# Two fused expert layers behind a gated scan: the second layer of chunks 0 and 1 joined into one stage at the end

## The chip, the cores and the metric

The kernel runs on one core of one Trainium2 chip. The metric is the device time of one execution in microseconds; the median of several runs counts. TensorE does the matrix products, ScalarE (ACT) and VectorE (DVE) the element-wise work on fp32 tiles, GpSimd (POOL) more of it, and SyncE (SP) issues the DMAs.

## What is computed

6080 tokens of 256 features run through a gated recurrence and then through two feed-forward layers, in fp32 (x is the scan's output for the first, and the first layer's output for the second):

```python
f = lower_bound + (1.0 - lower_bound) * sigmoid(f_logit)
for t in range(S):                      # the scan
    h = f[:, t] * h + (1 - f[:, t]) * x[:, t]
    y[:, t] = h
h = x @ w_in0                           # 256 -> 2048
x = (h * sigmoid(1.702 * h)) @ w_out0   # 2048 -> 256
h = x @ w_in1
g = where(h >= 1, h, where(h <= -1, 0, (h + 1) ** 2 / 4))
out = g @ w_out1
```

## The kernel before

**Precision.** Each fp32 product is made of three fp32r matmuls: every operand is split into a high part (a rounded copy, made by ScalarE: the functions with `_hi`) and the remainder (a subtraction, made by VectorE or GpSimd: `_lo`), and high x high, high x low and low x high are added up in PSUM (`three`, L566). A matmul has a 128 x 128 stationary operand and a moving one of `width(si)` columns (tokens).

**Stages.** Tokens are cut into seven chunks (L18); a stage `(l, c)` is layer l over chunk c, and the stages run one after another in the order of `STAGES` (L26): (0,0) (0,1) (1,0) (0,2) (1,1) (0,3) (1,2) (0,4) (1,3) and so on to (0,6) (1,5) (1,6), numbered by `si` from 0. Chunks 0 and 1, of 448 and 512 tokens, are plain: 16 tiles (one of 128 hidden features each), and for each tile 6 matmuls up into a hidden bank and 6 down into two accumulators (`unit`, L599, called for d = 0 and 1), so 192 matmuls a stage. Chunks 2 to 6 have 1024 tokens, two times 512, and use a fast scheme with seven block products in place of eight for the first matrix of a layer: 8 groups a stage, each with 7 products of 3 matmuls of 512 columns and 4 units of 6 matmuls, so 45 matmuls (`group`, L702). Between the products of a chain ScalarE takes snapshots of the bank (`take`, L870), which TensorE waits for (s_snap), and VectorE adds them to other banks (`evac`, L1195). Down products of a tile come three tiles (or about a group) behind its up products, so the element-wise work on a tile has about 5 us of slack.

**Inputs of a stage.** A seven-product stage needs seven input tiles (B11, B21, B22, T1, T3, T2, T4; `x_hi`, `x_lo`), among them sums of the others (`t_sum` on VectorE for layer 0, `z_sum` on GpSimd for layer 1). They are made during the stage before. For layer 0 they come from the scan of the chunk (`sigmoid_step` and `f_step` on ScalarE, `drive_step` and `scan_step` on VectorE, in four quarters), whose gate and state are loaded by `load_gate` and `load_state`, 1024 KB each.

**Weights.** The up weights of a layer are split once, in the first stage that uses them (`blocks_hi`, `blocks_lo`), stored in DRAM (`keep_blocks`) and loaded for each later group by `load_weights` (L451), two groups ahead; a seven-product group also needs four sums of blocks (`weight_sums`, `sums_hi`, `sums_lo`, `keep_sums`; job 0 to 7 for layer 0, 8 to 15 for layer 1; where each is made is said by `SUMS_AT`, L185). Its load is three DMAs of 256, 512 and 128 KB, and TensorE waits for all three before the group's first product. The down weights are split once and stay in SBUF (`down_hi`, `down_lo`); their raw form comes through small buffers in zraw, by `load_raw_down`, which waits until the buffer's last user is done.

**Order.** Every engine runs its own program, written out by hand: `plain_fill(si, s)` names the extra work at tile s of a plain stage, `fill(si, g, place)` that in a group. SyncE's program (L514) is one queue: whatever stands behind a waiting instruction waits too.

## Time and profile before

| | us |
|---|---|
| median of 3 runs (1017.29 to 1018.53) | 1017.85 |
| the profiled execution | 1017.41 |
| its span, first to last instruction | 1015.6 |
| TensorE busy | 1007.3 |
| ScalarE busy | 705.0 |
| VectorE busy | 687.6 |
| GpSimd busy | 579.4 |

The span is shorter than the execution's time by what lies around the first and the last instruction. A matmul's row shows how long it was in the pipeline (0.39 us for 512 columns), and the next one begins before it ends: the pitch from start to start is what counts. DMAs are issued by SyncE's queue, and "to landing" is the time from issue to the last byte's signal.

### The profile page before, as it was taken

Reading aid. Unit: us, or ns where it says so; the run is one execution under the profiler, and the core shown is the slowest. Engines: PE = TensorE matmul, PEld = TensorE weight load, DVE = VectorE, ACT = ScalarE, POOL = GpSimd, SP = SyncE. Lnnn points to the kernel's source line nnn. Section 1 sums busy time; section 2 is a strip of 40 time slices with the busy share of each in tenths; the row PEclk is TensorE's granted clock in tenths of the full one; section 3 lists DMA queues with packets and bytes.
Section 4 is the critical chain, followed back from the end, with each engine's and each line's share of the span. In section 5 each row is a group of like instructions: output and inputs, shape, how many; then the busy total and the mean of one; then the engine's idle time right before and its main releaser. Section 6 shows DMA issues by size and latency. Waiting matters only on the chain.

```text
span 1015.6 us, 14155 instructions
## 1 busy us (share of the span) xinstructions
PE 1007.3 (99%) x4401; PEld 821.6 (81%) x4401; DVE 687.6 (68%) x959; ACT 705.0 (69%) x1305; POOL 579.4 (57%) x471
## 2 busy tenths in 40 slices
PE   8999999999999999999999999999999999999998
PEld 6988988888888888888888888888888888888886
DVE  7764766665665786666677667678665546767666
ACT  7666767666766776677677676667766667777665
POOL 4577768756677364456647346745635664673432
PEclk9999999999999999999999999999999999999999
DMA  9766564436523232532223333232324222232421
GB/s 314 249 239 208 178 245 157 145 130 217 192 96 107 73 109 73 179 128 77 106 73 109 145 108 127 83 100 73 109 73 147 77 84 99 73 110 73 149 75 42
DMA packets 53212, 130.76 MB, mean 129 GB/s; under 512 B 6032, under 2 KB 16912, under 8 KB 52112
## 3 DMA queue, kind: packets, MB, share of 16 engines
q1 hardware_dynamic: 52992, 129.85, 36.8%
q8 instruction: 35, 0.57, 0.2%
q14 instruction: 41, 0.34, 0.1%
q10 hardware_dynamic: 144, 0.00, 0.0%
HBM read 106.82 MB, written 23.00 MB: 128 GB/s over the span
## 4 chain that ended last, share of the span: by engine, by line
PE 98%; DVE 0%; DMA 0%; POOL 0%; issue 0%; ACT 0%; SPq 0%; DVEq 0%; POOLq 0%
PE chain L568 26%; PE acc L623 17%; PE acc L620 17%; PE acc L619 17%; PE pair L568 13%; PE single L568 7%; DMA state<-x_dram 0%; POOL w_down0lo L1403 0%; DVE acc L1132 0%; DVE state L1113 0%; SPq L495 0%; ACT xin0hi L802 0%; DVE zout L1192 0%; ACT w_down0hi L852 0%; DVE acc L1098 0%
## 5 line engine op out<-in xcount | busy, mean ns | idle before, releaser
L1443 POOL TENSOR_TENSOR g_lo<-g_act,g_hi 128x512 fp32r<-128x512 f32 (+1 forms) x269 | 355.0, 1321 | 397.0 <-ACT g_hi L915 392.0
L875 ACT ACTIVATE spare<-chain 128x512 f32<-128x512 f32 x240 | 143.3, 597 | 189.5 <-PE chain L568 189.0
L1204 DVE TENSOR_TENSOR spare<-pair,spare 128x512 f32<-128x512 f32 x160 | 110.6, 691 | 181.9 <-PE pair L568 181.5
L915 ACT ACTIVATE g_hi<-g_act 128x512 fp32r<-128x512 f32 (+1 forms) x269 | 168.1, 625 | 5.4 <-DVE g_act L1228 3.4
L568 PE MATMUL chain<-xin1hi,w_main 128*128 128x512 f32 x416 | 162.6, 395 | 0.0
L623 PE MATMUL acc<-g_lo,w_down0hi 128*128 128x512 f32 (+1 forms) x384 | 150.2, 391 | 0.0
L619 PE MATMUL acc<-g_hi,w_down0hi 128*128 128x512 f32 (+1 forms) x384 | 149.8, 390 | 0.3 <-POOL w_down0lo L1403 0.3
L623 PE MATMUL acc<-g_lo,w_down1hi 128*128 128x512 f32 (+1 forms) x384 | 150.0, 391 | 0.0
L620 PE MATMUL acc<-g_hi,w_down1lo 128*128 128x512 f32 (+1 forms) x384 | 149.9, 390 | 0.0
L620 PE MATMUL acc<-g_hi,w_down0lo 128*128 128x512 f32 (+1 forms) x384 | 149.9, 390 | 0.0
L619 PE MATMUL acc<-g_hi,w_down1hi 128*128 128x512 f32 (+1 forms) x384 | 149.7, 390 | 0.0
L568 PE MATMUL chain<-xin0hi,w_main 128*128 128x512 f32 (+2 forms) x360 | 134.5, 385 | 0.1
L908 ACT ACTIVATE g_act<-g_act,one_half 128x512 f32<-128x512 f32 (+1 forms) x96 | 68.7, 716 | 63.4 <-DVE g_act L1215 63.4
L1204 DVE TENSOR_TENSOR single<-single,spare 128x512 f32<-128x512 f32 x80 | 55.7, 697 | 60.0 <-PE single L568 59.6
L568 PEld LDWEIGHTS chain<-xin1hi,w_main 128*128 128x128 f32 x416 | 78.1, 188 | 18.4 <-DMA w_a<-blocks_kept 0.3
L619 PEld LDWEIGHTS acc<-g_hi,w_down0hi 128*128 128x128 f32 x384 | 72.0, 188 | 16.9 <-POOL w_down0lo L1403 0.4
L619 PEld LDWEIGHTS acc<-g_hi,w_down1hi 128*128 128x128 f32 x384 | 72.1, 188 | 16.7
L620 PEld LDWEIGHTS acc<-g_hi,w_down1lo 128*128 128x128 f32 x384 | 72.0, 188 | 16.7
L620 PEld LDWEIGHTS acc<-g_hi,w_down0lo 128*128 128x128 f32 x384 | 72.0, 188 | 16.5
L623 PEld LDWEIGHTS acc<-g_lo,w_down0hi 128*128 128x128 f32 x384 | 72.1, 188 | 16.1 <-DVE g_lo L1239 0.3
L623 PEld LDWEIGHTS acc<-g_lo,w_down1hi 128*128 128x128 f32 x384 | 72.1, 188 | 15.6
L568 PE MATMUL chain<-xin1lo,w_main 128*128 128x512 f32 x208 | 82.2, 395 | 0.0
(126 smaller groups left out, 1960.6 us busy)
## 6 DMA issues: line engine op xcount, KB each, us to landing
w_main<-sums_kept SPq DMA_DIRECT2D x80, 512.0 KB, 3.6
w_main<-blocks_kept SPq DMA_DIRECT2D x80, 256.0 KB, 2.8
w_a<-blocks_kept SPq DMA_DIRECT2D x80, 128.0 KB, 3.9
blocks_kept<-w_main SPq DMA_DIRECT2D x16, 512.0 KB, 4.3
w_main<-blocks_kept SPq DMA_DIRECT2D x16, 512.0 KB, 3.3
sums_kept<-xin0hi SPq DMA_DIRECT2D x16, 512.0 KB, 2.9
zout<-w_in_dram SPq DMA_DIRECT2D x24, 256.0 KB, 4.3
out_dram<-zout SPq DMA_DIRECT2D x10, 512.0 KB, 5.3
```

The source lines that it names most:

```text
L568: mm = pe.matmul(to, w[a], moving[b], start=start and i == 0, stop=stop and i == 2, skip_group_check=joined)
L619: pe.matmul(to, w[0], g_hi[i][:, 0:n], start=start, stop=False)
L620: pe.matmul(to, w[1], g_hi[i][:, 0:n], start=False, stop=False)
L623: pe.matmul(to, w[0], g_lo[i][:, 0:n], start=False, stop=stop).then_inc(s_unit, 1)
L875: act.activation(snap[k][:, 0:n], chain[g % 2][:, 0:n], ACT.Copy).then_inc(s_snap, 1)
L908: act.activation(t, t, ACT.Square, bias=one_half[:], scale=0.5).then_inc(s_t, 1)
L915: act.activation(g_hi[h % 4][:, 0:n], activated(h), ACT.Copy).then_inc(s_ghi, 1)
L1204: dve.tensor_tensor(to[:, 0:n], bank[:, 0:n], snap[(0, 2, 1)[k]][:, 0:n], ALU.add).then_inc(s_evac, 1)
L1443: pool.tensor_tensor(g_lo[h % 4][:, 0:n], g_act[h % 4][:, 0:n], g_hi[h % 4][:, 0:n].bitcast(F32), ALU.subtract).then_inc(s_glo_pool, 1)
```

## The change

The second layer of chunks 0 and 1 is no longer done in two plain stages (448 and 512 tokens, 384 matmuls). The 960 tokens are taken together as a chunk of two times 480, in seven products, and are the last stage, `(1, JOINED)`. The first layer's results for chunks 0 and 1 are stored in DRAM (`keep_z`) and loaded again one stage before the last (`load_z`).

The order of stages becomes (0,0) (0,1) (0,2) (0,3) (1,2) (0,4) (1,3) (0,5) (1,4) (0,6) (1,5) (1,6) (1,7): 13 stages, so that (0,2) follows (0,1) at once, and (0,3) follows (0,2). All inputs of (0,2) are made in stage 1 (ScalarE at tiles 7 to 13, GpSimd at `X_LO_AT`), and all eight `down_lo` of layer 1 too, by VectorE at `DOWN_AT`, where GpSimd did four of them. Since no plain stage of layer 1 is left, the blocks of layer 1 aren't made in place any more, but in jobs of their own ahead of the sums (`more_hi`, `more_lo`, `keep_more`), in stages 2, 3 and 4 (`SUMS_AT`: jobs 8 and 9 in groups 4 and 5 of stage 2, 10 and 11 in groups 0 and 1 of stage 3, 12 to 15 in groups 0 to 3 of stage 4). There they share one buffer, so each waits for the store of the one before. The sums' buffers move from xin0hi to zout and raw_more. TensorE waits for each input tile of a stage by itself instead of for the last of them, and in the first group after a plain stage the single product and a unit come before the second product of the chain. The core of the diff:

```diff
-WIDTH = (448, 512, 512, 512, 512, 512, 512)
-CHUNKS = len(WIDTH)
+WIDTH = (448, 512, 512, 512, 512, 512, 512, 480)
+CHUNKS, JOINED = 7, 7
 PLAIN = 2
 SPAN = [n if c < PLAIN else 2 * n for c, n in enumerate(WIDTH)]
 BASE = [K * P * sum(SPAN[:c]) for c in range(CHUNKS + 1)]
-assert sum(SPAN) == TOKENS
-STAGES = [(0, 0), (0, 1), (1, 0)]
-for _c in range(2, CHUNKS):
-    STAGES += [(0, _c), (1, _c - 1)]
-STAGES += [(1, CHUNKS - 1)]
+OUT_BASE = {c: 0 if c == JOINED else BASE[c] for c in (JOINED, *range(PLAIN, CHUNKS))}
+assert sum(SPAN[:CHUNKS]) == TOKENS and sum(SPAN[:PLAIN]) == SPAN[JOINED]
+STAGES = [(0, 0), (0, 1), (0, 2), (0, 3)]
+for _c in range(4, CHUNKS):
+    STAGES += [(1, _c - 2), (0, _c)]
+STAGES += [(1, CHUNKS - 2), (1, CHUNKS - 1), (1, JOINED)]
...
 for _g in range(4):
-    SUMS_AT[1, 4 * _g + 1] = _g
-for _g in range(3):
-    SUMS_AT[4, 2 * _g + 1] = NG + 3 + _g
-for _g in range(7):
-    SUMS_AT[3, _g] = 4 + _g
+    SUMS_AT[1, 3 * _g + 1] = _g
+    SUMS_AT[2, _g] = 4 + _g
+    SUMS_AT[4, _g] = NG + 4 + _g
 for _g in range(2):
-    SUMS_AT[5, _g] = 2 * NG - 2 + _g
+    SUMS_AT[2, 4 + _g] = NG + _g
+    SUMS_AT[3, _g] = NG + 2 + _g
+LATE = {3: 1, 5: 0, 7: 0}
+X_LO_AT = (8, 9, 11, 12, 13, 14, 15)
+DOWN_AT = (0, 2, 4, 6, 8, 13, 14, 15)
...
+        z_kept = nc.dram_tensor("z_kept", (P, K, SPAN[JOINED]), F32, kind="Internal").ap()
...
-        made_sums = [xin[0][0][:, 2 + 2 * r:4 + 2 * r, :].rearrange("p a b -> p (a b)") for r in range(2)]
+        made_sums = [zout[:, 0:1024].bitcast(F32R), raw_more[:].bitcast(F32R)]
...
+                if SUMS_AT.get((4, job - NG - 4)) == job and job < NG + 6:
+                    sp.wait_ge(s_xlo, input_n(4, 6))
...
+            def keep_more(job):
+                sp.wait_ge(s_more, job - NG + 1)
+                sp.dma_start(blocks[job], made_sums[0].bitcast(F32)).then_inc(s_kept_blocks[job - NG], 16)
+            def keep_z(si):
+                n, m = WIDTH[si], 2 * BANK[si]
+                for d in range(K):
+                    sp.wait_ge(s_z[d], evac_n(si, 0))
+                begin = sum(WIDTH[:si])
+                sp.dma_start(z_kept[:, :, begin:begin + n], zraw[:, m * n:(m + K) * n].rearrange("p (d n) -> p d n", d=K))\
...
+            def load_z():
+                n = WIDTH[JOINED]
+                sp.wait_ge(s_z_kept, 32)
+                sp.wait_ge(s_xlo, input_n(NS - 2, 6))
+                for t in range(2):
+                    sp.dma_start(zraw[:, t * K * n:(t + 1) * K * n].rearrange("p (d n) -> p d n", d=K),
+                                 z_kept[:, :, t * n:(t + 1) * n]).then_inc(s_z_back, 16)
...
-                    if g in (2, 4, 6):
-                        load_raw_down(1, g // 2 + 1)
-                    if g in (4, 5):
-                        load_raw_up(1, 2 * (g - 4))
-                        load_raw_up(1, 2 * (g - 4) + 1)
-                if si == 2:
-                    keep_blocks(1, g)
-                    if g + 4 < NG:
-                        load_raw_up(1, g + 4)
-                    if g in (0, 1, 5):
-                        load_raw_down(1, (5, 6, 0, 0, 0, 7)[g])
+                    if g < 5:
+                        load_raw_down(1, g + 2)
+                    if g == 5:
+                        keep_z(0)
+                    if g == 6:
+                        load_raw_down(1, 7)
+                        load_gate(3)
+                if (si, g) == (2, 0):
+                    load_state(3)
+                if (si, g) == (2, 2):
+                    keep_z(1)
+                if (si, g) == (3, 0):
+                    load_gate(4)
+                    load_state(4)
+                if (si, g) == (3, 7):
+                    load_raw_sums(12)
+                    load_raw_sums(13)
+                if (si, g) == (NS - 2, 0):
+                    load_z()
                 if not is_plain(si):
+                    if SUMS_AT.get((si, g), 0) >= NG:
+                        keep_more(SUMS_AT[si, g])
                     kept(si, g)
...
+                if g == 0:
+                    pe.wait_ge(s_xlo, input_n(si, xs))
...
+                if si == 4 and start and d == 0:
+                    pe.wait_ge(s_down_dve, down_made(1, NG - 1)[1])
...
+                if after_plain and g == 0:
+                    half_unit(second, 0)
                 pe.wait_ge(s_snap, third_n(S, 0))
                 product(si, g, S2, T2, c, False).then_inc(s_chain, 1)
-                half_unit(second, 0)
-                if first is not None:
-                    single_product(si, g)
+                if not (after_plain and g == 0):
+                    half_unit(second, 0)
+                    if first is not None:
+                        single_product(si, g)
...
+            def more_hi(job):
+                act.wait_ge(s_raw_sums[job % 2], 16 * (job // 2 + 1))
+                if job == NG:
+                    act.wait_ge(s_kept_sums[NG - 2], 16)
+                else:
+                    act.wait_ge(s_kept_blocks[job - NG - 1], 32)
+                act.activation(made_sums[0].rearrange("p (a b f) -> p a b f", a=4, b=2)[:, :, 0, :],
+                               raw_sums[job % 2].rearrange("p (a f) -> p a f", a=4), ACT.Copy).then_inc(s_more_hi, 1)
...
+                if job < 2:
+                    blocks_made(act, NG - 1)
+                elif job < NG:
+                    act.wait_ge(s_kept_sums[job - 2], 16)
+                elif job == NG:
+                    act.wait_ge(s_kept_sums[NG - 1], 16)
+                else:
+                    act.wait_ge(s_kept_sums[job - NG - 1], 32)
...
+                    act.wait_ge(s_tsum, tsum_n(si, T4))
+                    act.wait_ge(s_xlo, input_n(si, (T1, T3, T2)[k]))
...
+                    if s == 7:
+                        z_evac(0, 0)
+                    for j in {7: (B11,), 8: (B21,), 10: (B22,), 11: (T1,), 12: (T3, T2), 13: (T4,)}.get(s, ()):
+                        x_hi(2, j)
+                    if s in DOWN_AT:
+                        down_hi(1, DOWN_AT.index(s))
...
+                if SUMS_AT.get(following, 0) >= NG:
+                    more_hi(SUMS_AT[following])
...
+            def more_lo(job):
+                dve.wait_ge(s_more_hi, job - NG + 1)
+                made = made_sums[0].rearrange("p (a b f) -> p a b f", a=4, b=2)
+                dve.tensor_tensor(made[:, :, 1, :], raw_sums[job % 2].rearrange("p (a f) -> p a f", a=4),
+                                  made[:, :, 0, :].bitcast(F32), ALU.subtract).then_inc(s_more, 1)
...
+                    if s in (6, 8):
+                        drive_step(2, 2 + s // 8)
+                    if s == 9:
                         last_scan(2)
-                    if s in (7, 8):
-                        direct_lo(s - 7)
-                if si == 2:
-                    if s == 4:
-                        z_evac(1, 0)
-                    if s in (3, 5, 7):
-                        t_sum(3, s // 2 - 1)
-                    if s in (1, 8, 10, 12):
-                        down_lo(1, {1: 4, 8: 5, 10: 6, 12: 7}[s])
-                if si == 4:
-                    if s == 1:
-                        last_scan(3)
-                    if s in (3, 4):
-                        z_evac(3, s - 3)
-                    if s in (8, 10, 12):
-                        t_sum(5, (s - 8) // 2)
+                    if 10 <= s <= 12:
+                        t_sum(2, s - 10)
+                    if s in DOWN_AT:
+                        down_lo(1, DOWN_AT.index(s))
...
+                if place == 0 and SUMS_AT.get((si, g), 0) >= NG:
+                    more_lo(SUMS_AT[si, g])
+                if si == 2:
+                    if 1 <= g <= 4 and place == 0:
+                        drive_step(3, g - 1)
+                    if 1 <= g <= 3 and place == 2:
+                        scan_step(3, g - 1)
+                    if (g, place) == (4, 2):
+                        last_scan(3)
+                    if (g, place) in ((4, 3), (5, 0), (5, 2)):
+                        t_sum(3, {(4, 3): 0, (5, 0): 1, (5, 2): 2}[g, place])
...
+                    if late and (g, place) == (0, 3):
+                        drive_step(c, 3)
+                    if (g, place) == (late, 1):
+                        last_scan(c)
...
+                    if STAGES[si][1] == JOINED:
+                        pool.wait_ge(s_z_back, 32)
+                    else:
+                        for d in range(K):
+                            pool.wait_ge(s_z[d], evac_n(STAGES.index((0, STAGES[si][1])), 1))
+                    if si == 4:
+                        pool.wait_ge(s_kept_blocks[SUMS_AT[3, 1] - NG], 32)
+                    else:
+                        pool.wait_ge(s_store, stored_n(si - 2))
...
+                    if s in X_LO_AT:
+                        x_lo(2, X_LO_AT.index(s))
...
```

## Rows read from the trace of the kernel before

**Rows 1.** The page: busy us, share, instructions; then the granted clock in 40 slices.
```profile
PE 1007.3 (99%) x4401; PEld 821.6 (81%) x4401; DVE 687.6 (68%) x959; ACT 705.0 (69%) x1305; POOL 579.4 (57%) x471
...
PEclk9999999999999999999999999999999999999999
```

**Rows 2.** The chain that ended last: start us, us, what; TensorE's first products of tiles and groups.
```profile
18.33 1.23 PE chain L568 x6
...
42.77 1.23 PE pair L568 x6
...
77.92 1.38 PE single L568 x6
...
80.68 1.37 PE chain L568 x6
...
88.98 1.23 PE single L568 x6
...
294.24 0.71 PE chain L568 x3
...
315.12 0.71 PE chain L568 x3
```

**Rows 3.** The timeline of SyncE in stage 1: start us, us, engine, line, what.
```profile
76.56 0.33 SPq L458 DMA_DIRECT2D w_main<-blocks_kept  x1
```

**Rows 4.** The timeline of ScalarE and of VectorE at tile 12 of stage 1.
```profile
79.82 0.62 ACT L915 ACTIVATE g_hi<-g_act 128x512 fp32r<-128x512 f32 x1
...
79.96 0.70 DVE L1222 SCALAR_TENSOR_TENSOR single<-g_act,single 128x512 f32<-128x512 f32 x1 [1.48 <-ACT g_act L901]
```

**Rows 5.** Groups by shape: line, engine, op, out<-in, count | busy us, mean ns | idle before.
```profile
L1113 DVE SCALAR_TENSOR_TENSOR state<-gate,state 128x512 f32<-128x512 f32 x20 | 20.9, 1044 | 0.0
...
L1132 DVE TENSOR_TENSOR_SCAN state<-gate,state 128x512 f32<-128x512 f32 x10 | 15.1, 1511 | 0.0
...
L1184 DVE TENSOR_TENSOR w_down1lo<-zraw,w_down1hi 128x512 fp32r<-128x512 f32 x4 | 5.1, 1273 | 0.6 <-ACT w_down1hi L852 0.6
...
L1170 DVE TENSOR_TENSOR spare<-state 128x1024 f32<-128x1024 f32 x2 | 2.8, 1424 | 0.0
```

**Rows 6.** The timeline of VectorE and of GpSimd (POOL) at tile 7 of stage 1.
```profile
63.97 2.32 DVE L1132 TENSOR_TENSOR_SCAN state<-gate,state 128x512 f32<-128x512 f32 x1
...
63.92 1.28 POOL L1443 TENSOR_TENSOR g_lo<-g_act,g_hi 128x512 fp32r<-128x512 f32 x1 [0.29 <-ACT g_hi L915]
```

**Rows 7.** Windows: us, then busy us of PE, PEld, DVE, ACT, POOL, granted clock, DMA share, GB/s.
```profile
116.00:119.00 3.00, 3.00 (x16) 2.76 (x16) 2.56 (x4) 1.72 (x5) 2.88 (x3) 1.00 0.89 369
61.32:88.98 27.66, 27.66 (x121) 22.52 (x121) 16.81 (x24) 16.26 (x31) 21.09 (x21) 1.00 0.55 188
...
367.17:377.60 10.43, 10.43 (x47) 8.45 (x46) 10.01 (x12) 8.13 (x17) 7.38 (x6) 1.00 0.24 87
```

**Rows 8.** SyncE's issues, and landing of the gate (issued 112.83) and state (issued 131.20) loads.
```profile
111.89 0.33 SPq L434 DMA_DIRECT2D blocks_kept<-w_main  x1
...
DMA to landing us min/median/max: 5.9/5.9/5.9
...
129.82 0.32 SPq L461 DMA_DIRECT2D w_main<-blocks_kept  x1
...
DMA to landing us min/median/max: 7.5/7.5/7.5
```

**Rows 9.** Timelines of VectorE and ScalarE in group 2 of a seven-product stage of layer 1.
```profile
359.01 0.69 DVE L1204 TENSOR_TENSOR spare<-pair,spare 128x512 f32<-128x512 f32 x1 [1.48 <-PE pair L568]
...
363.19 0.60 ACT L875 ACTIVATE spare<-chain 128x512 f32<-128x512 f32 x1 [1.09 <-PE chain L568]
...
366.55 0.72 ACT L908 ACTIVATE g_act<-g_act,one_half 128x512 f32<-128x512 f32 x1 [0.72 <-DVE g_act L1215]
```

**Rows 10.** The timeline of TensorE in the head; in brackets its idle time before.
```profile
3.37 3.71 PE L760 MATMUL pair<-warm 128*128 128x512 bf16 x9 [3.37 <-ACT gate L788]
7.86 0.37 PE L568 MATMUL single<-xin0hi,w_main 128*128 128x224 f32 x1 [0.78 <-POOL w_main L1380]
```

More of the change, by code:

```diff
@@ L691, in plain_stage @@
                         first_up(1, s).then_inc(s_up, 1)
-                    if before is False and s < 4:
-                        for d in range(K):
-                            unit(h0 - 4 + s, d)
-                    elif before and s < LAG:
+                    if si == 1 and s < LAG:
                         for d in range(K):
@@ L1409, in x_lo @@
                 if plain:
[L1410 removed]
+                    tile = column(source, 2 + j, n)
                 else:
```

364 lines of the change are left out of this document (136 added, 228 removed).

## The prediction

> **What bounds the kernel now.** First the page's busy shares and slices: TensorE is busy for 1007.3 of 1015.6 us, and the granted clock is at nine tenths or more in every slice [rows 1]. Then the chain of work that ended last: behind the head it is made of matmuls, and the same step recurs at a fixed pitch: 24.44 us for ten tiles of 12 matmuls in a plain stage of 448 tokens, 11.06 us for four in one of 512, and 20.88 us for two groups (90 matmuls) in a seven-product stage [rows 2]. Last the waits of TensorE itself: 3.37 and 0.78 us in the head [rows 10], and beyond that only tenths. So time is the number of matmuls times their pitch, plus head and tail, and a part of the change counts if it alters that number, or if it makes a wait on TensorE where there is none.
>
> **The change, part by part.** All sums are made against the profiled execution, 1017.41 us with a span of 1015.6; it lies 0.44 under the median of 1017.85, which is inside the spread of the three runs.
>
> *Matmuls removed.* A plain stage has 16 tiles of 12 matmuls, a seven-product stage 8 groups of 45. Per matmul the pitches are 24.44/120 = 0.2037 us (448 columns), 11.06/48 = 0.2304 (512) and 20.88/90 = 0.232 (512, seven products) [rows 2]; 64 columns cost 0.0267 us, so 0.42 ns each, and 480 columns in a seven-product stage cost 0.232 - 32 x 0.00042 = 0.2186. Out go 192 x 0.2037 = 39.11 and 192 x 0.2304 = 44.24 us, in come 360 x 0.2186 = 78.70. That is 83.35 - 78.70 = 4.65, or **4.7 us** (5.1 if the 480-column matmul takes the plain stage's overhead). The moved stages keep their matmuls. Nothing at the old boundaries is saved, since no boundary had an idle TensorE. The last evacuation and store are 480 wide instead of 512: under 0.1 us, left out.
>
> *The new third stage waits for its weights.* This is the largest cost. In stage 1 tiles 12 and 13 begin at 77.92 and 80.68, tiles 14 and 15 follow at the same pitch, and the next stage's first matmul stands at 88.98 [rows 2]. Stages 0 and 1 keep their matmuls, so this is when (0,2) wants its weights. In the new order SyncE, at group 6 of stage 1, first issues load_raw_down(1, 7), which waits until VectorE has done down_lo(1, 5) at tile 13, since they share a buffer; then load_gate(3), 1024 KB; and only then the 896 KB of the first group's weights. SyncE gets to group 6 just after it has issued the weights for group 7, which it did at 76.56 [rows 3]; nothing else holds it up before.
> When does down_lo(1, 5) end? ScalarE begins the copy behind tile 12's tanh at 79.82 and takes 0.62 us [rows 4]; x_hi(2, T4) and down_hi(1, 5) follow at 0.5 to 0.6 us each, so the copy is there at about 81.5, and the subtraction takes 1.27 us [rows 5]: 82.8 at the earliest. It can't be much earlier, since on VectorE it is behind tile 12's gate step of 79.96 to 80.66 [rows 4]. It can be later: VectorE gets, in tiles 6 to 12 (19.4 us), seven gate steps and four remainders of 0.7, two drives of 1.04, two down_lo of 1.27, two scans of 1.5 to 2.3, and three T sums, of which the double one takes 1.42 and the single ones, taken as two thirds to all of it, 1.0 to 1.4 [rows 5, 6]: 18.7 to 21.2 us. And there the two engines hinder each other: a scan, 1.5 us in the mean, took 2.32 beside a GpSimd subtraction that had begun 0.05 before it and took 1.28 [rows 6]. GpSimd, busy for 21.1 of 27.7 us in that stretch [rows 7], gets seven x_lo where it had three down_lo and a blocks_lo. I take 84.0, between 82.8 and 85.5.
> How long do the transfers take? In a like case 512, 256 and 1024 KB were issued at 111.89, 112.44 and 112.83, and the last landed 5.9 us after its issue, so 6.8 us for 1792 KB [rows 8], while the DMA engines moved up to 369 GB/s [rows 7]. Here 256, 1024 and 896 KB stand in the queue: 384 KB more, 1.1 us: 8.0. In another case 896 KB and then 1024 KB took from 129.82 to 131.2 + 7.5 = 138.7, 8.9 us for 1920 KB, which with the 256 KB more gives 9.6 here [rows 8]. I take 8.4, nearer to the first, where nothing else was queued. So the weights land at 84.0 + 8.4 = 92.4 against 88.98: **3.4 us** of idle TensorE (bounds 82.8 + 8.0 and 85.5 + 9.6: 1.8 to 6.1). Should GpSimd be late with a remainder in stage 1, TensorE waits there instead and this wait shrinks by as much, so I don't add it.
> The slowdown of VectorE beside GpSimd is stated by the Trainium skill (SBUF — State Buffer, "Who interferes with whom"): whichever of the two starts first on the shared port pair holds it for its whole instruction. The 2.32 us scan agrees. By that rule taken strictly, the seven x_lo and VectorE's operations with two SBUF inputs would add up end to end in stage 1, and the wait would be near its upper bound.
>
> *Weights of layer 1 made in stages 2 to 4.* Per job ScalarE gets one more copy (0.6), VectorE a subtraction of about 1.27, SyncE a 512 KB store. The room in a layer-1 group: ScalarE waits 1.09 us ahead of its third snapshot, and behind it 0.72 for VectorE [rows 9]. Between the product that a snapshot follows and the product that needs it TensorE has two or three others of 3 matmuls, 1.4 to 2.1 us, of which the snapshot takes 0.6; so ScalarE may be about 1 us late at a snapshot before TensorE feels it. VectorE has a hole of 1.48 us behind a group's first gate step [rows 9], just where more_lo is put; but in group 3 of a layer-1 stage it is busy for 10.0 of 10.4 us [rows 7], and in stage 4 it now gets more_lo in each of groups 0 to 3, and in group 1 the last scan. I expect 0.3 us there (0 to 2). In stage 2, group 4, VectorE has more_lo, a drive, a scan and a T sum beside the regular work: by the same durations over 11 us of work in 10.44, spread over two groups: 0.2 (0 to 1). At the start of stage 3 the gate and state of chunk 4, 2048 KB, are issued ahead of the store of keep_more(10), which more_hi(11) waits for on ScalarE: at the rate above it lands about 11 us into a group of 10.44, and ScalarE's takes of group 1 stand behind that wait: 0.4 (0 to 1.5). Together **0.9** (0 to 4); not below nothing, since TensorE doesn't idle there now.
>
> *Free edits.* Storing z of chunks 0 and 1 and reloading it (four transfers of about 0.5 MB) lies in stages 1, 2 and 11; the reload is issued at the start of the stage before its use, where a group's stretch moves 87 GB/s [rows 7]. The direct copies from the accumulator go; they were hidden. Eight groups of blocks are no longer made in place in (1,0). Uncovered, each would cost under 1 us. The end has three layer-1 stages in a row; the inputs of the last are made in the same places as before, with the store of two stages back as the only new wait of GpSimd, which it has in every mid stage.
>
> **Sum.** 1017.41 - 4.7 + 3.4 + 0.9 = 1017.0.
>
> **Rivals.**
> (B) *The gain arrives.* The wait for weights is at its lower bound or under it, and the rest is absorbed: 1017.41 - 4.7 + 1.8 = 1014.5; down to 1012.7 if there is no wait at all. For: the slack of about 5 us between a tile and its second-layer unit, which hid all such work so far. Against: the queue order can't be undone by a quick engine, since the copy and the subtraction of tile 13 stand behind tile 12.
> (C) *The clock falls in the wait.* The idle time is long, 5 us, and the granted clock drops to 1.2 GHz for a stretch. The nine first matmuls, after an idle head of 3.37 us, took 3.71 us for 9 x 512 columns [rows 10], 0.41 us each, the pace of 1.2 GHz (the granted clock in the slices is too coarse to show it [rows 1]), against 0.23 later: that costs 3.71 - 9 x 0.23 = 1.6 us. 1017.41 - 4.7 + 5.0 + 0.9 + 1.6 = 1020.2. It is slower than before from a total loss of 4.7 us, and measurably so from 6.8. For: VectorE and GpSimd hold each other up in the very tiles that gate the load. Against: a wait of 0.78 us in the head was followed by the full pace (224 columns every 0.11 us), so only a long wait can do it [rows 10].
> The Trainium skill says the same of long gaps (TensorE: Matmul & The Clock Gate, "HAM oscillation"): a DMA wait that is long enough sends the clock back to half, and it is paid anew at each such wait. No stretch of this trace after the head shows it.
> (D) *The joined stage doesn't run at TensorE's pace*, because fixed costs of the other engines don't shrink with 480 columns: 0.1 us per group, 1017.8. Against: ScalarE is busy for 8.1 of 10.4 us in such a group, and VectorE's 10.0 hold T sums [rows 7] that the last stage lacks.
>
> **How the numbers follow.** Forecast 0.48 (1015.8 to 1019.5), B 0.29, C 0.18, D and what I don't see 0.05. A measurement can tell about 0.2%, 2.0 us, from no change: that is under 1015.8 or over 1019.9. B gives faster 0.29; C and the upper edge of the forecast and D slower 0.23; the rest 0.48. The range of 8 in 10 takes in most of B and of C: 1013.6 to 1020.8; the forecast's own is 1015.8 to 1019.5.
>
> **What would show it.** 4377 matmuls instead of 4401, the last stage's groups at about 9.84 us. At about 89 us one idle stretch of TensorE, ended by a DMA into w_main or w_a, whose issue stands behind that of gate, behind a wait of SyncE for w_down1lo. Short gaps before the snapshots' products in stages 2, 3 and 4. The forecast is wrong if TensorE goes through 89 us without a pause, or if a gap of over 1 us appears elsewhere.

## The result, and the profile after

The changed kernel takes **1028.67 us** (median of 5, 1027.53 to 1029.47), the one before 1017.85 beside it: a ratio of 1.0106, 95% interval 1.0091 to 1.0121. It is slower by 10.8 us, where the forecast was 1017.0 with a range that ended at 1020.8. The profiled execution took 1029.47, with a span of 1027.7 against 1015.6. (It is the longest of the five; the difference of its span, 12.1 us, is therefore 1.2 us more than that of the medians.)

The page of the changed kernel: busy us, share and instructions; the granted clock in 40 slices; and the shares of the chain that ended last.
```profile
PE 1010.1 (98%) x4377; PEld 819.5 (80%) x4377; DVE 707.4 (69%) x985; ACT 719.4 (70%) x1334; POOL 596.5 (58%) x476
...
PEclk9998999999999999999999999999999999999999
...
PE 88%; POOL 3%; DMA 3%; issue 2%; ACT 2%; DVE 1%; SPq 0%; ACTq 0%; DVEq 0%; POOLq 0%
```
The 24 matmuls are gone (4401 in [rows 1]). But the fourth slice of the clock shows an 8, and 12% of the chain now lie outside TensorE (2% before). Where it stood is read from TensorE's timeline: the first matmul behind each wait has its idle time in brackets.

TensorE's timeline in the changed kernel: start us, us, what, idle before and what ended it.
```profile
88.79 0.40 PE L676 MATMUL acc<-g_lo,w_down0hi 128*128 128x512 f32 x1
93.18 0.80 PE L617 MATMUL chain<-xin0hi,w_main 128*128 128x512 f32 x1 [4.00 <-DMA w_a<-blocks_kept]
93.78 0.63 PE L617 MATMUL chain<-xin0lo,w_main 128*128 128x512 f32 x1
94.20 0.63 PE L617 MATMUL chain<-xin0hi,w_main 128*128 128x512 f32 x1
...
139.78 0.64 PE L617 MATMUL chain<-xin0hi,w_main 128*128 128x512 f32 x1 [2.17 <-ACT spare L916]
140.21 0.63 PE L617 MATMUL chain<-xin0lo,w_main 128*128 128x512 f32 x1
...
194.41 0.50 PE L617 MATMUL chain<-xin1hi,w_main 128*128 128x512 f32 x1 [0.54 <-ACT spare L916]
...
197.64 0.51 PE L672 MATMUL acc<-g_hi,w_down0hi 128*128 128x512 f32 x1 [0.58 <-DVE zraw L1215]
...
302.89 0.50 PE L617 MATMUL chain<-xin0hi,w_main 128*128 128x512 f32 x1 [1.35 <-ACT spare L916]
...
957.83 0.37 PE L617 MATMUL chain<-xin0hi,w_main 128*128 128x480 f32 x1
...
967.66 0.38 PE L617 MATMUL chain<-xin0hi,w_main 128*128 128x480 f32 x1
...
977.49 0.37 PE L617 MATMUL chain<-xin0hi,w_main 128*128 128x480 f32 x1
```
Behind the waits of 4.00 and 2.17 us the matmuls begin 0.43 us apart, not 0.23: that is the half clock (1.2 GHz). Windows of the same kernel show it beside what the DMA engines moved.

Windows: us, then busy us of PE, PEld, DVE, ACT, POOL, granted clock, DMA share, GB/s.
```profile
92.20:99.03 6.83, 5.85 (x14) 4.60 (x15) 0.32 (x1) 1.11 (x2) 2.81 (x5) 0.50 1.00 406
99.10:105.00 5.90, 5.90 (x25) 4.48 (x25) 1.84 (x4) 4.14 (x8) 0.14 (x1) 1.00 0.00 0
...
139.99:143.40 3.41, 3.41 (x9) 2.66 (x9) 3.41 (x4) 0.74 (x2) 3.41 (x3) 0.50 0.39 155
```
The account of the span. A gap's loss is the distance between the starts of the two matmuls around it less the usual pitch; the clock's is 0.2 us for each matmul in a half-clock stretch (14 and some 8 of them, at 0.427 against 0.232; in the first 1.0 of the 6.8 us TensorE was still idle).

| where | us |
|---|---|
| matmuls removed | -4.7 |
| start of stage 2, at 89 to 93: idle | +4.1 |
| the half clock behind it, 6.8 us of it | +2.7 |
| stage 2, at 137 to 140: idle | +2.3 |
| the half clock behind it, 3.4 us of it | +1.6 |
| start of stage 3, at 194 to 198: four small gaps | +1.9 |
| stage 4, at 282 to 314: gaps of 0.6, 0.65, 1.6 and 0.7 | +3.6 |
| small ones at 85, 101, 136 and 144 | +1.1 |
| sum (measured: 12.1) | +12.6 |

The mean granted clock of the profiled execution is 0.995, that of the four others 0.997 or 0.998, so they had less of the half clock than the table shows.

### The profile page after: what moved, and what is told of

It is laid out like the page before. It is cut to its first block, busy times and chain, and to the rows that moved or that the text cites. A ratio compares the mean times of both kernels' runs of the same rounds, so it can differ in the third digit from the quotient of the medians.

```text
span 1027.7 us, 14282 instructions
## 1 busy us (share of the span) xinstructions
PE 1010.1 (98%) x4377; PEld 819.5 (80%) x4377; DVE 707.4 (69%) x985; ACT 719.4 (70%) x1334; POOL 596.5 (58%) x476
## 4 chain that ended last, share of the span: by engine, by line
PE 88%; POOL 3%; DMA 3%; issue 2%; ACT 2%; DVE 1%; SPq 0%; ACTq 0%; DVEq 0%; POOLq 0%
PE chain L617 24%; PE acc L676 16%; PE acc L672 16%; PE acc L673 16%; PE pair L617 11%; PE single L617 6%; DMA blocks_kept<-zout 1%; POOL g_lo L1470 1%; DMA zout<-w_in_dram 1%; DMA w_a<-blocks_kept 1%; POOL xin1lo L1438 1%; ACT g_hi L956 0%; POOL raw_more L1418 0%; POOL xin0lo L1438 0%; DVE zout L1182 0%
## 5 line engine op out<-in xcount | busy, mean ns | idle before, releaser
L1470 POOL TENSOR_TENSOR g_lo<-g_act,g_hi 128x512 fp32r<-128x512 f32 (+2 forms) x277 | 367.9, 1330 | 400.9 <-ACT g_hi L956 392.4
L916 ACT ACTIVATE spare<-chain 128x512 f32<-128x512 f32 (+1 forms) x264 | 156.8, 594 | 203.5 <-PE chain L617 196.7
L1227 DVE TENSOR_TENSOR spare<-pair,spare 128x512 f32<-128x512 f32 (+1 forms) x176 | 120.9, 687 | 185.6 <-PE pair L617 185.3
L956 ACT ACTIVATE g_hi<-g_act 128x512 fp32r<-128x512 f32 (+2 forms) x277 | 172.9, 624 | 4.2 <-DVE g_act L1251 3.3
L617 PE MATMUL chain<-xin0hi,w_main 128*128 128x512 f32 (+3 forms) x424 | 163.8, 390 | 8.2 <-DMA w_a<-blocks_kept 4.0
L617 PE MATMUL chain<-xin1hi,w_main 128*128 128x512 f32 x352 | 137.8, 395 | 0.5 <-ACT spare L916 0.5
L1227 DVE TENSOR_TENSOR single<-single,spare 128x512 f32<-128x512 f32 (+1 forms) x88 | 61.1, 695 | 69.8 <-PE single L617 69.6
L617 PEld LDWEIGHTS chain<-xin0hi,w_main 128*128 128x128 f32 x424 | 80.0, 189 | 27.2 <-ACT spare L916 5.7
L1238 DVE TENSOR_SCALAR g_act<-spare 128x512 f32<-128x512 f32 (+1 forms) x96 | 87.1, 907 | 3.3
```

What stands on the lines that cost most here:

```text
L617: mm = pe.matmul(to, w[a], moving[b], start=start and i == 0, stop=stop and i == 2, skip_group_check=joined)
L916: act.activation(snap[k][:, 0:n], chain[g % 2][:, 0:n], ACT.Copy).then_inc(s_snap, 1)
L956: act.activation(g_hi[h % 4][:, 0:n], activated(h), ACT.Copy).then_inc(s_ghi, 1)
L1227: dve.tensor_tensor(to[:, 0:n], bank[:, 0:n], snap[(0, 2, 1)[k]][:, 0:n], ALU.add).then_inc(s_evac, 1)
L1238: dve.tensor_scalar(g_act[i][:, 0:n], hidden_of(h), -1.0, 1.0, ALU.max, ALU.min).then_inc(s_clip, 1)
L1470: pool.tensor_tensor(g_lo[h % 4][:, 0:n], g_act[h % 4][:, 0:n], g_hi[h % 4][:, 0:n].bitcast(F32), ALU.subtract).then_inc(s_glo_pool, 1)
```

## The first wait: what stands in the queue of SyncE

The theory of the prediction (Q below): the wait at 89 is set by the order of SyncE's queue, since the first weights of stage 2 stand behind `load_raw_down(1, 7)`, which waits for VectorE, and behind the 1024 KB of `load_gate(3)`. The rival (V): VectorE, ScalarE and GpSimd have so much to do in stages 1 and 2 that TensorE would wait for them anyway. SyncE's issues in the changed kernel:
```profile
76.44 0.56 SPq L499 DMA_DIRECT2D w_main<-blocks_kept  x1
84.04 0.34 SPq L440 DMA_DIRECT2D zraw<-w_out_dram  x1
84.43 0.42 SPq L408 DMA_DIRECT2D gate<-f_logit_dram  x1
84.96 0.36 SPq L502 DMA_DIRECT2D w_main<-blocks_kept  x1
85.37 0.43 SPq L504 DMA_DIRECT2D w_main<-sums_kept  x1
85.84 0.60 SPq L508 DMA_DIRECT2D w_a<-blocks_kept  x1
```
SyncE stands still from 77 to 84.04, and the last of the three weight transfers (`w_a`, 7.3 us from issue to landing) is there at 93.14.

**Both loads out of the way.** They go behind the weights:
```diff
-                    if g == 6:
-                        load_raw_down(1, 7)
-                        load_gate(3)
...
                 if G + 2 < GROUPS and not is_made(G + 2):
                     load_weights(G + 2)
+                if (si, g) == (1, 6):
+                    load_raw_down(1, 7)
+                    load_gate(3)
```

> At group 6 of stage 1 SyncE issues the 896 KB of weights for (0,2) first, and load_raw_down(1, 7) and load_gate(3) behind them. Theory Q (the queue's order makes the wait): the weights are issued at about 82.2 us and land by 86, the idle 4.1 us at 93 us goes, and with it the fall of the clock behind it (3.4 us): 1028.7 - 7.5 = 1021.2. Rival V (ScalarE, VectorE and GpSimd are late in stage 1 and TensorE would wait for their input tiles in any case): the gap only changes its releaser, at least 3 us of it stay, and the clock may still fall: 1025 or more. The gaps at 140, 194 and 282 to 314 us stay in both.

Measured: median 1025.34 (4 runs, ratio 1.0062, 1.0041 to 1.0083), the profiled execution 1022.02 with a span of 1020.2, 7.5 less than 1027.7, as Q says. The gap of 4.1 us became two, 0.6 at 92 to 95 and 0.6 at 103, and no clock fell in that trace. But the three other executions took 2.7 to 4.6 us longer than the profiled one, at mean granted clocks of 0.998 and 0.999, and the median is only 3.3 us under that of the changed kernel, inside V's range. What those executions lost isn't shown. So it is the trace that speaks for Q here, not the median; two kernels that differ in this wait alone follow below (`e10_first_wait`).

**One at a time.** `e2_gate_behind` moves `load_gate(3)` alone, `e3_raw_behind` `load_raw_down(1, 7)` alone.

> Only load_gate(3) goes behind the weights; the wait for down_lo(1, 5) stays ahead. Q, with both causes needed: the weights are issued at 84.5 and land 4.5 to 5 us later, at 89 to 89.5, so the gap shrinks to 0.5 us and the clock stays up: 7 us off a profiled execution of about 1028. If the wait for VectorE alone is the cause, over 2 us of the gap stay; by V at least 3.

> Only load_raw_down(1, 7) goes behind the weights; the 1024 KB of gate stay ahead. Q, with both causes needed: nothing holds SyncE up, gate is issued at about 77 and the weights at 82.2, landing by 86.5: no gap at 93 us, no fall of the clock there, 7.5 us less. If the bytes alone are the cause, over 2 us of the gap stay; by V at least 3.

Measured: 1025.17 (span 1023.4) and 1022.31 (span 1020.5), one execution each, so that only their traces are read. With the gate behind, TensorE still waits for weights, but shortly:
```profile
91.59 0.50 PE L618 MATMUL chain<-xin0hi,w_main 128*128 128x512 f32 x1 [0.96 <-DMA w_a<-blocks_kept]
```
With the raw block behind, it doesn't wait at all between 88 and 94 (0.27 us at 94.5, 0.58 at 103). So the whole gap needs VectorE's wait: without it the 1024 KB cost nothing, since the gate load is then issued at 77.92, 4.5 us ahead of the weights. While that wait stands, the 1024 KB make up about 2.9 of the 4.1 us, and 1.2 stay without them.

## Stages 2 and 3: the engine that waits in order

In stage 2 ScalarE comes late to the snapshot that TensorE needs at 139.78. ScalarE's timeline in the changed kernel, there and at the start of stage 3:
```profile
134.46 0.63 ACT L894 ACTIVATE raw_more<-zout 128x512 fp32r<-128x512 f32 x1 [2.40 <-POOL zout L1413]
136.97 0.63 ACT L874 ACTIVATE zout<-zout 128x512 fp32r<-128x512 f32 x1 [1.88 <-DMA zout<-w_in_dram]
...
139.15 0.57 ACT L916 ACTIVATE spare<-chain 128x512 f32<-128x512 f32 x1
...
192.21 0.63 ACT L874 ACTIVATE zout<-zout 128x512 fp32r<-128x512 f32 x1 [3.14 <-DMA blocks_kept<-zout]
...
193.79 0.58 ACT L916 ACTIVATE spare<-chain 128x512 f32<-128x512 f32 x1
```
L874 is `more_hi`, L916 a snapshot. At 137 `more_hi(8)` waits for its raw load, which was issued only at 131.98; the snapshot stands behind it. At 192 `more_hi(11)` waits for the store of job 10, issued at 182.08 behind 2048 KB, 10.0 us from issue to landing. Two edits, first both together, on top of the first experiment:
```diff
-    SUMS_AT[2, 4 + _g] = NG + _g
+    SUMS_AT[2, 5 + _g] = NG + _g
...
-                if (si, g) == (3, 0):
-                    load_gate(4)
-                    load_state(4)
                 if not is_plain(si):
                     if SUMS_AT.get((si, g), 0) >= NG:
                         keep_more(SUMS_AT[si, g])
                     kept(si, g)
+                if (si, g) == (3, 0):
+                    load_gate(4)
+                    load_state(4)
```

> Three moves together: weights first as in e1; jobs 8 and 9 one group later (groups 5 and 6 of stage 2), so that the raw weights of each have landed before the copy that needs them; and at the start of stage 3 the store of keep_more(10) ahead of load_gate(4) and load_state(4). If ScalarE's waits for DMAs are the cause of the gaps at 140 us (2.3 us, and 1.7 for the clock) and 194 us (1.95), these go as well: 1028.7 - 7.5 - 4.0 - 1.9 = 1015.3. If they come from too much work on VectorE, GpSimd and ScalarE there, the same gaps turn up one group later, and the time stays at 1019 or more.

Measured: median 1017.80 (10 runs, ratio 0.9999, 0.9989 to 1.0008), span 1016.3. The gaps in stage 2 and at 190 are gone, with nothing left of either. What is left: 1.35 us at 92 to 95, 0.6 at 103, and 3.5 in stage 4. The median is 2.5 us above the 1015.3 that was expected. Against `e1_weights_first` it is 7.5 us less, where the spans differ by 3.9: again what the usual execution of that kernel lost isn't shown.

Each alone, on the changed kernel, so with the first wait still in it:

> The changed kernel with one edit: the first two weight jobs of layer 1 (8 and 9) in groups 5 and 6 of stage 2, not 4 and 5. In its trace ScalarE waited 1.88 us for the raw load of job 8 and 2.40 for the sums in group 4, TensorE lost 2.3 us at 139.8 and the granted clock was half for 3.4 us. If that load's place is the cause, this gap and this fall of the clock go (about 4 us less span, 1023.7) and the gaps at 93 and 194 stay; if the work of jobs 8 and 9 is just too much for stage 2, the gap moves one group on.

> The changed kernel with one edit: at the start of stage 3 the store of job 10 is issued ahead of the gate and state of chunk 4 (2048 KB). In its trace the store took 10.05 us from issue to landing, ScalarE waited for it until 192.2, and TensorE lost 1.95 us at 194 to 198. If what is in flight ahead of the store is the cause, that gap goes to under 0.3 us and the span falls by 1.7 to 2.0, with the gaps at 93 and 140 as they were. If two splits, two sums and their remainders in two groups are the cause, at least 1 us of it stays.

Measured: 1025.82 (span 1024.0) and 1024.77 (span 1023.0), one execution each. With the jobs later the gap at 140 and its half clock are gone, and 1.4 of the 1.9 us at 190 stay. With the store first the gaps at 194 are gone, and in stage 2 1.0 and 1.6 us are lost at 137 and 141, but the clock stays up there. Its span fell by 4.7 us, of which only the 1.9 at 194 are the edit's; most of the rest is that the half clock lasted 3.4 us behind the first wait, not 6.8, and didn't come at 140. Each edit removes its own gap, and neither gap moved on to another group.

The trace of `e5_store_first`, whose stage 2 is that of the changed kernel, shows a second cause there. ScalarE waited for the raw load for only 0.20 us, and still TensorE was idle for 0.49 and 1.37. The second time the snapshot waited for VectorE, which had `more_lo` (L1182) and a drive step (L1134) ahead of the addition (L1227) that ScalarE needed:
```profile
136.66 1.78 DVE L1182 TENSOR_TENSOR zout<-zout 128x512 fp32r<-128x512 f32 x1
138.37 1.78 DVE L1134 SCALAR_TENSOR_TENSOR state<-gate,state 128x512 f32<-128x512 f32 x1
140.07 0.68 DVE L1227 TENSOR_TENSOR spare<-pair,spare 128x512 f32<-128x512 f32 x1
...
140.84 0.60 ACT L916 ACTIVATE spare<-chain 128x512 f32<-128x512 f32 x1 [2.81 <-DVE spare L1227]
```
The traces of e1, e2 and e3 have the same wait of 2.81 us and 1.36 to 1.38 us of idle TensorE behind it. `e4_jobs_later` takes the jobs away from the late load and from the drive steps at once, so how much each does isn't shown.

**The first wait alone.** `e8_gate_ahead` (next section) has neither of these two faults nor the first wait; this kernel puts only the two loads at (1, 6) back:

> The kernel of e8_gate_ahead with the one first thing put back as the change has it: load_raw_down(1, 7) and load_gate(3) both ahead of the first weights of stage 2 at (1, 6). It gives the cost of that wait alone. By the trace of the changed kernel: TensorE idle for 4.1 us at 89 to 93, then 6.8 us at half the granted clock, which costs 3.4 us. So 7.5 us over e8_gate_ahead, median about 1023.5, if idle time and clock add up; about 4 us over it if the half clock was a property of that one execution, or if work that was late anyway catches up in the wait.

Measured: 1023.91 (4 runs, ratio 1.0061, 1.0046 to 1.0076) against 1017.65 for `e8_gate_ahead`: 6.3 us. In the traces it is 5.6 us: an idle time of 4.12 where there was a gap of 0.6, and a half-clock stretch, but one of 3.4 us, as in `e4_jobs_later` and `e5_store_first`, not of 6.8. Windows of this kernel:
```profile
88.00:93.60 5.60, 1.48 (x7) 0.87 (x6) 2.15 (x3) 1.09 (x2) 3.30 (x3) 1.00 0.97 305
...
94.14:97.55 3.41, 3.41 (x10) 2.63 (x9) 0.00 (x0) 1.11 (x2) 1.72 (x3) 0.50 1.07 425
```
So the clock's share of this wait is 1.5 us in three traces and 2.7 in the one of the changed kernel. It differs between executions: the mean granted clock of this kernel's four was 0.998, 0.996, 0.998 and 0.996. The 7.5 us expected had taken half of the 6.8 us for the loss, 3.4.

## Stage 4: too much work, or one buffer?

First the gate load goes back ahead of the weights, as in `e3_raw_behind`, since in `e7_three` VectorE and ScalarE waited 4.8 us for the last raw block, queued with the weights and the gate:
```profile
90.78 0.63 ACT L880 ACTIVATE w_down1hi<-zraw 128x512 fp32r<-128x512 f32 x1 [4.75 <-DMA zraw<-w_out_dram]
```

> The kernel of e7_three with load_gate(3) put ahead of the weights again (only load_raw_down(1, 7) stays behind them), and everything else as in e7_three. In the trace of e7_three the last raw block of layer 1 was issued at 84.20 and landed at 90.76, VectorE and ScalarE waited 4.8 us for it, and TensorE lost 1.35 us at 92 to 95 and 0.58 at 103. In e3_raw_behind, where the gate stood ahead, there was no gap there. Theory Q (the queue's order and what is in flight decide): these 1.9 us go, span 1014.4, median about 1016.0, faster than before by 1 to 3 us. Theory V (the vector engines are overloaded in stage 1 and 2 and would make TensorE wait anyway): the gap stays above 1 us and the median is 1017.5 or more.

Measured: 1017.65 (10 runs, ratio 1.0003, 0.9994 to 1.0013), span 1015.7. In the trace the 1.9 us became 0.64, as Q says, but the median didn't follow (1016.0 expected) and stayed in V's range; against the kernel before, e7 and e8 can't be told apart.

Then stage 4, on this kernel. It holds 2.85 us of gaps at 285 to 302 and 0.6 at 270. By theory M the cause is the split that was moved there, `more_hi` and `more_lo`; by theory P it is the order of GpSimd's work. `e6_no_split_4` leaves out the split of jobs 12 to 15 and keeps their stores and loads:

> The kernel of e8_gate_ahead, and the split of the blocks of jobs 12 to 15 is left out: more_hi (ScalarE) and more_lo (VectorE) don't run in stage 4, and keep_more stores what is in the buffer, so the stores and loads of SyncE stay as they are. These are the four operations pairs that were moved there. Theory M (the added split is what makes TensorE wait in stage 4): the gaps at 270, 286 to 291 and 300 to 303, 3.5 us in e7_three, go down to under 0.8 us, the span falls by about 3. Theory P (GpSimd is what is late there: weight sums, remainders of the sums and the inputs of stage 5 in the same groups, and the store of the sums behind it that ScalarE waits for): the gaps at 286 to 291 keep at least 1.5 of their 2.2 us, the span falls by under 1.5.

Measured: 1016.36 (span 1014.6). The gap at 270 went, but of the 2.85 us 2.6 stayed, and ScalarE waited longer, for something else:
```profile
286.28 0.63 ACT L895 ACTIVATE raw_more<-zout 128x512 fp32r<-128x512 f32 x1 [2.98 <-DMA sums_kept<-raw_more]
```
L895 is `sums_hi(13)`: it writes the only buffer for layer 1's sums, and waits until those of job 12 are stored out of it. GpSimd's order decides when that is; in the same kernel it does a 2.28 us `x_lo` (L1439) and then the remainder of job 12 (L1419), with SyncE's store behind it:
```profile
279.27 2.28 POOL L1439 TENSOR_TENSOR xin1lo<-state,xin1hi 128x512 fp32r<-128x512 f32 x1
281.52 1.75 POOL L1419 TENSOR_TENSOR raw_more<-zout,raw_more 128x512 fp32r<-128x512 f32 x1
```
So `x_lo` alone is moved, and in another kernel everything that makes stage 5's inputs:
```diff
                 else:
+                    a = g - (si == 4)
-                    if place == 0 and 2 <= g <= 4:
-                        x_lo(si + 1, (B11, B22, T3)[g - 2])
+                    if place == 0 and 2 <= a <= 4:
+                        x_lo(si + 1, (B11, B22, T3)[a - 2])
...
```

> The kernel of e8_gate_ahead with GpSimd's x_lo for stage 5 alone one group later (groups 3 to 6 of stage 4); the scan, the T sums of VectorE and the x_hi of ScalarE stay where they are. Nothing is left out. In e8_gate_ahead TensorE lost 2.85 us at 285 to 302, in e9_inputs_later 0.39. In the trace of e6_no_split_4 ScalarE stood 2.98 us ahead of the split of the sums of job 13, for the store of job 12 out of the only buffer, which GpSimd had finished only behind a 2.28 us x_lo. Theory P (GpSimd's order is the cause): the 2.85 us go down to under 1.0 and ScalarE's wait ahead of the sums' split to under 0.8. Theory of VectorE and ScalarE (their T sums, scan and copies are the cause): at least 2 us stay.

> The kernel of e8_gate_ahead, and in stage 4 the work for the inputs of stage 5 is one group later: last_scan at (2, 1), the three T sums at (3, 3), (4, 1), (4, 3) in place of (2, 1), (2, 3), (3, 1), the x_hi of ScalarE and the x_lo of GpSimd in groups 2 to 6 in place of 1 to 5. Nothing is left out. Groups 0 to 3 hold the weight jobs 12 to 15, so the two kinds of work overlap less. Theory of too much work at once in groups 1 to 3 of stage 4 (whichever engine): the gaps at 286 to 303 (2.9 us in e7_three) go down to under 1 us; span about 1012.5, median about 1014, faster than before by 3 to 5 us. If it is the single job chain itself (split, sums, remainder, store, next job) that is late, whatever lies beside it, they stay.

Measured: `e11_gpsimd_later` 1016.20 (span 1014.4), with 1.24 of the 2.85 us left. ScalarE's split of job 13 doesn't wait at all any more, while 1.0 us of waiting for the store stays at another job:
```profile
285.59 0.62 ACT L895 ACTIVATE raw_more<-zout 128x512 fp32r<-128x512 f32 x1
```
`e9_inputs_later`: median 1015.79 (10 runs, ratio 0.9981, 0.9971 to 0.9991), span 1014.6, 0.4 us left of the 2.85 and 0.66 at 271. So GpSimd's order makes up 1.6 of the 2.85 us, a little less than theory P asked for, and the T sums, the scan and the copies of VectorE and ScalarE 0.85 (seen only on top of GpSimd's); the split itself is worth 0.3 there and the 0.6 at 270.

In the medians `e9_inputs_later` is 1.6 us faster than the kernel before, where 3 to 5 were expected, and 1.9 faster than `e8_gate_ahead`. Its span is only 1.1 us under that of `e8_gate_ahead`, though 2.4 us of gaps are gone. The head hides the rest: in this execution the first products began 0.21 us apart, and 0.11 only from 11.84 on, where `e8_gate_ahead` has 0.11 from 7.66 on.
```profile
8.43 0.42 PE L618 MATMUL single<-xin0lo,w_main 128*128 128x224 f32 x1
8.65 0.42 PE L618 MATMUL single<-xin0hi,w_main 128*128 128x224 f32 x1
...
11.84 0.28 PE L618 MATMUL pair<-xin0hi,w_main 128*128 128x224 f32 x1
11.95 0.27 PE L618 MATMUL chain<-xin0hi,w_main 128*128 128x224 f32 x1
```
The 394th matmul begins at 89.35 here and at 87.88 in `e8_gate_ahead`, 1.5 us apart, and the edit doesn't touch the head. So spans of single executions can differ by as much for another reason; the gaps in a trace say more.

**Two more moves**, each for a gap whose late instruction had been read from the trace:
```diff
-DOWN_AT = (0, 2, 4, 6, 8, 13, 14, 15)
+DOWN_AT = (0, 2, 4, 6, 8, 13, 14)
...
+                    if g == 0:
+                        down_hi(1, 7)
...
+                    if (g, place) == (0, 3):
+                        down_lo(1, 7)
...
-                    if late and (g, place) == (0, 3):
+                    if late and (g, place) == ((1, 3) if si == 4 else (0, 3)):
                         drive_step(c, 3)
```

> The kernel of e9_inputs_later with two more moves. First: the last raw block of layer 1 is split one stage step later, down_hi(1, 7) in group 0 of stage 2 and down_lo(1, 7) behind its last gate step, not at tile 15 of stage 1, where VectorE waited 3.17 us for its load and the gate steps stood behind that (TensorE lost 0.63 us at 94 to 96). Second: in stage 4 the drive step of chunk 4 is at (1, 3), not at (0, 3), so that more_lo(13) and the second evacuation of z begin 0.7 us earlier (TensorE lost 0.66 us at 271, released by the DVE write of zraw). Nothing is left out. Expected by the theory that each gap is set by what stands ahead of the late instruction on its own engine: both gaps go to 0.1 or less, 1.2 us, median about 1014.6, faster than before by 2 to 4 us. If VectorE is short of time as a whole there, the gaps come back within two groups, and the median stays at 1015.8.

Measured: 1015.55 (11 runs, ratio 0.9984, 0.9975 to 0.9993); span 1013.2. A miss: the gap at 92 to 96 fell from 0.63 to 0.27, but one of 0.9 came at 102.65, and the one at 270 stayed at 0.66. VectorE's timeline shows what stood there:
```profile
97.72 0.69 DVE L1210 TENSOR_TENSOR w_down1lo<-zraw,w_down1hi 128x512 fp32r<-128x512 f32 x1
98.32 0.68 DVE L1250 SCALAR_TENSOR_TENSOR g_act<-g_act,spare 128x512 f32<-128x512 f32 x1
98.92 1.79 DVE L1139 SCALAR_TENSOR_TENSOR state<-gate,state 128x512 f32<-128x512 f32 x1
```
The postponed subtraction (L1210) pushes a drive step (L1139), which takes 1.79 us here, and the evacuation that ScalarE's next snapshot waits for comes behind both. Only 0.6 us of that are the added work. The same drive step took 0.69 us in `e9_inputs_later`, where it began 0.03 us before a GpSimd subtraction; in `e12_two_more` it began 0.37 us behind one. First GpSimd's row in `e12_two_more`, then the drive step and GpSimd's row in `e9_inputs_later`:
```profile
98.55 3.33 POOL L1481 TENSOR_TENSOR g_lo<-g_act,g_hi 128x512 fp32r<-128x512 f32 x2 [4.16 <-ACT g_hi L957]
...
100.50 0.69 DVE L1137 SCALAR_TENSOR_TENSOR state<-gate,state 128x512 f32<-128x512 f32 x1
...
100.53 3.07 POOL L1477 TENSOR_TENSOR g_lo<-g_act,g_hi 128x512 fp32r<-128x512 f32 x2 [2.99 <-ACT g_hi L957]
```
So VectorE is short of time here, as V says, but more by GpSimd's work beside it than by its own. In `e9_inputs_later` and `e12_two_more` the intervals lie under 1: they are faster than the kernel before by 1.6 to 1.9 us of the 4.7 that the removed matmuls are worth, and can't be told apart from each other.

## Why the prediction was wrong, step by step

*Matmuls removed, -4.7.* Right. A group of the joined stage takes 967.66 - 957.83 = 9.83 us, the next one 9.83 (9.84 foreseen), and there are 4377. (The 5.1 us that the prediction gives in brackets comes to 5.2.) Rival D, a joined stage off TensorE's pace, is out.

*The wait for weights, +3.4.* Place, cause and size right. `down_lo(1, 5)` was taken to end at 84.0, and SyncE goes on at 84.04. That is partly luck: the 1.2 us over the earliest, 82.8, were put to VectorE being busy, and VectorE stood idle; it was ScalarE's copy ahead that ended at 82.68 and not at 81.5. The transfers were taken at 8.4 us and needed 9.1; the idle time was 4.1, inside 1.8 to 6.1. The rule of the Trainium skill (SBUF — State Buffer, "Who interferes with whom"), taken strictly, was to put the wait near its upper bound; it didn't come to that.

*The clock.* Here a step failed. The fall was made a rival that needs "a total loss" of 5 us of idle time, on the ground that 0.78 us had not done it and "only a long wait can do it" [rows 10]. Between 0.78 and 3.37 us the trace of before showed nothing, and the forecast's own wait of 3.4 us lay at the upper end of that hole. The 0.78 us were weak evidence besides: in `e9_inputs_later` the same place of the head has a wait of 0.62 us, and there the products behind it ran at half pace until 11.84. The granted clock fell in that wait, and again behind 2.17 us: 2.7 + 1.6 = 4.3 us in the profiled run. The price per fall was right in kind (1.6 foreseen, 1.5 to 2.7 seen); its condition and its chance of 0.18 were not. The section "HAM oscillation" of the Trainium skill (TensorE: Matmul & The Clock Gate), that a long DMA wait sends the clock back to half, agrees with the wait of 4.00 us and with those of 4.12, 4.14 and 4.49 in e10, e5 and e4. The second fall stood behind a wait for ScalarE, not for a DMA, and is seen in this one trace; the same fault gave two shorter waits in four others (e1, e2, e3, e5), and no fall.

*Weights of layer 1 made in stages 2 to 4, +0.9 (0 to 4).* The largest miss: 2.3 + 1.9 + 3.6 = 7.8 us, and 1.6 for the clock on top. The step priced the added **work** against the free time of each engine. Most of the waits came from what the added instructions themselves **wait for**, on an engine that works in order and has a snapshot behind them; the rest from VectorE's operations, which take longer beside GpSimd's:
- Stage 2, 0.2 foreseen, 2.3 seen: ScalarE stood 2.40 us for GpSimd's sums and 1.88 for a raw load. The step looked at VectorE only; `e4_jobs_later` removes the gap without removing any work. VectorE's part was underpriced too: it took `more_lo` at 1.27 and a drive at 1.04, and both took 1.78, which in four other traces makes a gap of 1.4 of its own.
- Stage 3, 0.4 foreseen, 1.9 seen: the wait for the store was found, and its landing foreseen at 11 us into the group (10.0 us from issue seen). Only its effect was underpriced; `e5_store_first` removes the gap.
- Stage 4, 0.3 foreseen, 3.6 seen: the single buffer of the sums was not looked at, and the room on GpSimd not counted. `more_lo`, taken at 1.27 us from [rows 5], has a median of 1.78. (1.27 wasn't a price of the operation alone: behind it stand four of 1.08 to 1.38 us, each begun 0.47 to 0.76 us behind a GpSimd operation.)

The prediction's own sign of being wrong, a gap of over 1 us elsewhere, came twice: 2.17 at 140 and 1.35 at 303.

*Free edits, 0.* Right: no gap lies at the store and reload of z or at the boundaries of the last stages; behind 314 TensorE waits for nothing that the account shows.

*The range.* Its upper end was the idle clock rival alone, 1020.8. Even with the bound of 4 for the weight jobs and that rival together, 1017.41 - 4.7 + 5.0 + 4 + 1.6 = 1023.3, it would have ended 5 us short. The parts of the weight jobs add up to 4.5, not 4, and beside the store in stage 3 (0 to 1.5) none had a term for a wait on a transfer or on a buffer.

In medians against before the steps are +10.8 for the change, +6.5 with the jobs later and the store first (so 4.3 for those two), +0.2 without the first wait (6.3), -1.6 with stage 5's inputs later (1.9). Taken in the other order they come out otherwise: 3.3 for the first wait (`e1_weights_first`) and then 7.5 for the other two (`e7_three`). So the sum of the three faults is measured, about 10.8, but the share of each depends on what else is in the kernel. The 3 us that are left to the full -4.7 are, by the traces, small gaps in stages 1 to 4 and differences in the head; which of them could be had without a new one is open.

## What to carry to other kernels

When work is moved onto an engine that runs in order, list for each added instruction what it waits for (a load, a store out of the only buffer, another engine), when that is issued and behind how many bytes, and which instruction that the bottleneck needs stands behind it; free time of the engine says little. Price a VectorE subtraction as it runs beside GpSimd, not by the mean of its group. In an issuing queue nothing that waits goes ahead of a transfer that is due soon, and a large load that isn't due yet goes behind it, unless it can be issued much earlier. Price an idle stretch of TensorE above the longest that the trace shows to be harmless with the clock's fall in it, in the forecast and not in a rival.

## What the runs showed of the hardware that wasn't expected

- The granted clock fell behind idle times of 4.00 and 2.17 us in the changed kernel, of 4.12 in `e10_first_wait`, and of 4.14 and 4.49 in `e5_store_first` and `e4_jobs_later`; behind 1.39 in `e2_gate_behind`, 1.37 in `e5_store_first` and 1.12 in `e8_gate_ahead` it stayed up. After nearly the same wait the half-clock stretch was once 6.8 us long and three times 3.4.
- The same VectorE subtraction of 512 columns, `more_lo`, took 1.77 to 1.80 us seven times, each time with a GpSimd operation that had begun 0.03 to 0.51 us before it, and 0.68 us the one time without. Its row by line (duration ns min/median/max), and the timelines of VectorE and GpSimd for one of either kind, in the changed kernel:
```profile
L1182 DVE TENSOR_TENSOR zout<-zout x8: 680/1780/1797, 139.4 to 302.0; 128x512 fp32r<-128x512 f32 x8
...
265.87 1.79 DVE L1182 TENSOR_TENSOR zout<-zout 128x512 fp32r<-128x512 f32 x1
...
265.83 1.28 POOL L1470 TENSOR_TENSOR g_lo<-g_act,g_hi 128x512 fp32r<-128x512 f32 x1 [0.87 <-ACT g_hi L956]
...
151.48 0.68 DVE L1182 TENSOR_TENSOR zout<-zout 128x512 fp32r<-128x512 f32 x1
```
  What is left of GpSimd's operation, 1.24 us, and 0.55 more make up the 1.79: here the rule of the Trainium skill cited in the prediction, that the first holds the port for its whole instruction, agrees. The four behind the mean of 1.27 in [rows 5] fit as well: GpSimd's operation still had 0.53 to 0.83 us to go when they began, and they took 1.08 to 1.38.
- The store of job 10 (512 KB) took 10.0 us from issue to landing behind 2048 KB of loads, against 2.6 in the median of the eight such stores.
- The head of the same program isn't the same in every execution: the first products began 0.21 us apart up to 11.84 us in `e9_inputs_later`, and 0.11 apart from 7.66 on in `e8_gate_ahead`.
